# Spreading the decay rows by matmuls for four units of a gated attention, gate rows in three parts, and the exponents of two units ahead of the first product

## The reference

```python
for t in range(S):
    m_new = np.maximum(f_gate[:, :, t] + m, i_gate[:, :, t])
    f_stab = np.exp(f_gate[:, :, t] + m - m_new)
    i_stab = np.exp(i_gate[:, :, t] - m_new)
    C = f_stab * C + i_stab * outer(v_t, k_t);  n = f_stab * n + i_stab * k_t
    y[:, :, t] = sigmoid(o_t) * (C @ q_t) / np.maximum(np.abs(n @ q_t), 1.0)
x = y as (2, 768, 320)
u = x + (relu(x.T @ w_tok1) @ w_tok2).T;  x = u + relu(u @ w_ch1) @ w_ch2
gate = sigmoid(causal convolution of x with 5 taps per channel)
out = (gate * (x @ w_val)) @ w_out
```

## Time and profile before

| what | value |
|---|---|
| runs | 309.8, 310.57, 307.46 us, median 309.8 |
| span of the profiled execution, first to last instruction | 308.2 us |
| what lies around the span, taken as median less span | 1.6 us |
| busy: TensorE, VectorE, ScalarE, GpSimd | 88%, 68%, 40%, 29% |
| mean granted clock of TensorE | 0.966 |

### The profile page before, as it was taken

The page is one execution under the profiler, slowest core; times in us unless marked ns, Lnnn a source line. Parts: engine busy times, 40 slices in busy tenths (PEclk is TensorE's granted clock), DMA queues, the critical chain, the costliest instruction groups (busy, mean ns, idle before and its releaser), DMA issues.

```text
span 308.2 us, 5374 instructions
## 1 busy us (share of the span) xinstructions
PE 270.8 (88%) x2024; PEld 258.5 (84%) x2024; DVE 210.7 (68%) x415; ACT 121.9 (40%) x224; POOL 89.4 (29%) x102
## 2 busy tenths in 40 slices
PE   0876765884999999999999999999999999999854
PEld 0765654783998999999899999999999999999754
DVE  7999999977778687576677740352774138763693
ACT  4344453432874453434434223323123333231623
POOL 4537445554046445334610400000004000040340
PEclk9999598796899999999999999999999999999999
DMA  7599833344547554242000001000000010000011
GB/s 223 158 309 310 241 128 83 100 170 144 169 128 217 141 155 117 66 136 65 2 0 0 3 0 66 0 0 2 0 2 1 32 34 0 2 0 1 23 43 64
DMA packets 26289, 25.70 MB, mean 83 GB/s; under 512 B 13976, under 2 KB 22008, under 8 KB 26264
## 3 DMA queue, kind: packets, MB, share of 16 engines
q1 hardware_dynamic: 21976, 18.72, 20.9%
q10 hardware_dynamic: 4288, 6.64, 6.5%
HBM read 23.34 MB, written 2.02 MB: 82 GB/s over the span
## 4 chain that ended last, share of the span: by engine, by line
PE 60%; DVE 17%; issue 7%; ACT 6%; DMA 4%; POOL 3%; SPq 1%; ACTq 0%; DVEq 0%; POOLq 0%
PE shared L1171 25%; PE h_ps L1309 18%; DVE prob L933 7%; PE s_ps L1209 3%; DVE gate L1037 2%; PE hv_ps L1190 2%; PE shared L1274 2%; PE s_ps L1246 2%; PE hv_ps L1194 2%; PE shared L1230 2%; DVE y_lo L942 1%; DMA G_all<-G_scratch 1%; PE shared L1259 1%; DMA stage<-val 1%; DMA stage<-wout 1%
## 5 line engine op out<-in xcount | busy, mean ns | idle before, releaser
L933 DVE SCALAR_TENSOR_TENSOR prob<-G_all,A_col,mask_sb 128x128 f32<-128x128 f32 x96 | 51.3, 602 | 0.2 <-DMA G_all<-G_scratch 0.2
L1101 DVE SCALAR_TENSOR_TENSOR h_lo<-shared,h_hi 128x384 fp32r<-128x384 f32 x48 | 26.5, 557 | 35.0 <-ACT h_hi L826 34.8
L1309 PE MATMUL h_ps<-ch_hi,h_hi 128*128 128x320 f32 x144 | 45.4, 315 | 0.0
L1309 PE MATMUL h_ps<-ch_hi,h_lo 128*128 128x320 f32 x144 | 44.5, 309 | 0.0
L826 ACT ACTIVATE h_hi<-shared 128x384 fp32r<-128x384 f32 x48 | 23.1, 488 | 53.8 <-PE shared L1171 50.8
L1309 PE MATMUL h_ps<-ch_lo,h_hi 128*128 128x320 f32 x144 | 44.3, 308 | 0.0
L697 ACT ACTIVATE prob<-prob 128x512 f32<-128x512 f32 x24 | 15.0, 631 | 48.5 <-DVE prob L933 48.4
L1171 PE MATMUL shared<-u_hi,ch_hi 128*128 128x384 f32 x96 | 32.9, 342 | 0.6 <-DVE yt L982 0.4
L1171 PE MATMUL shared<-u_lo,ch_hi 128*128 128x384 f32 x96 | 32.5, 339 | 0.0
L1171 PE MATMUL shared<-u_hi,ch_lo 128*128 128x384 f32 x96 | 32.5, 338 | 0.0
L1037 DVE SCALAR_TENSOR_TENSOR gate<-x,conv_sb,gate 128x384 f32<-128x384 f32 x44 | 29.0, 668 | 1.0
(11 more groups left out here) (189 smaller groups left out, 620.6 us busy)
## 6 DMA issues: line engine op xcount, KB each, us to landing
G_all<-G_scratch SPq DMA_DIRECT2D x11, 512.0 KB, 4.8
o_sig<-on ACTq DMA_DIRECT2D x2, 960.0 KB, 6.1
k_in<-kT SPq DMA_DIRECT2D x24, 80.0 KB
q_in<-qT SPq DMA_DIRECT2D x24, 80.0 KB
kn_in<-kn SPq DMA_DIRECT2D x12, 160.0 KB, 3.9
v_in<-vn SPq DMA_DIRECT2D x12, 160.0 KB, 4.6
stage<-ch ACTq DMA_DIRECT2D x3, 640.0 KB, 4.4
out<-o_sb SPq DMA_DIRECT2D x12, 160.0 KB, 1.8
```

What stands on the lines that cost most here:

```text
L933: last = dve.scalar_tensor_tensor(out=prob[(2 * u + g) % 4][:, tile_cols(j)], in0=G_all[u % 2][:, tile_cols(h)], scalar=A_col[:, col:col + ...
L1101: took(dve.scalar_tensor_tensor(out=h_lo[i % 3][:], in0=ps_of(key)[:, 0:T], scalar=0.0, in1=h_hi[i % 3][:].bitcast(F32), op0=ALU.max, op1= ...
L1309: last = pe.matmul(h2_ps[t][:, 0:DM], a[:, tile_cols(t)], w[:, f, :], start=(f == 0 and n == 0), stop=(f == FT - 1 and n == 2))
```

## The change

Four things are done together.
- `spread(u)` on TensorE: for units 0 to 3, a matmul per head whose weights are one column of the identity, repeated 128 times, and whose data are the 16 G rows, puts the head's G row on all 128 partitions of a bank of `h2_ps`. For units 1 to 3 eight more, 64 wide, put the rows for the decays in `h2_ps[2]`. Exponents and decays of these units read PSUM. Only units 4 to 11 still go through DRAM.
- From unit 4 on `h2_ps[2]` holds a copy of the mask; the exponents of units 4 to 6 read the mask from there and G from SBUF. Units 7 to 11 read both from SBUF as before.
- The gate rows are made in three parts, chunk 0, chunk 1, and chunks 2 to 5. The third stands behind the first product on VectorE.
- The exponents of unit 1 move ahead of the first product. The buffer for `ht` is doubled, fills of buffers change engine and place, and A and W columns are copied together by VectorE.

```diff
-ROWS_PARTS = ((0, 1), (1, NC))
+ROWS_PARTS = ((0, 1), (1, 2), (2, NC))
+SPREAD = 4
...
             sp.wait_ge(pool_init, 3)
             kn_chunk(0)
             v_chunk(0)
-            sp.wait_ge(G_saved[0], 16)
...
+            sp.wait_ge(zeroed_next, 2)
+            q_chunk(1)
             k_chunk(1)
-            q_chunk(1)
-            sp.wait_ge(G_saved[1], 32)
-            G_chunk(1)
             kn_chunk(1)
             v_chunk(1)
             piece(sp, 0)
             for u in range(2, NU):
                 chunk(u)
+                if u == 2:
+                    sp.wait_ge(G_ready, 3)
+                    G_save(sp, 0, SPREAD, NC, G_saved)
+                    G_save(sp, 1, 0, NC, G_saved)
...
+                if u < SPREAD:
+                    act.wait_ge(spread_ready, u + 1)
...
+                    act.activation(decay[:], h2_ps[2][:], ACT.Exp).then_inc(decay_ready, 1)
+                    if u == SPREAD - 1:
+                        act.wait_ge(decay_ready, with_state(u))
+                        act.activation(mask_ps, mask_sb[:], ACT.Copy).then_inc(mask_ready, 1)
+                    return
...
                         last = dve.scalar_tensor_tensor(
-                            out=prob[(2 * u + g) % 4][:, tile_cols(j)], in0=G_all[u % 2][:, tile_cols(h)],
-                            scalar=A_col[:, col:col + 1], in1=mask_sb[:], op0=ALU.add, op1=ALU.min)
+                            out=prob[(2 * u + g) % 4][:, tile_cols(j)],
+                            in0=h2_ps[g][:, tile_cols(j)] if u < SPREAD else G_all[u % 2][:, tile_cols(h)],
+                            scalar=A_col[:, col:col + 1], in1=mask_ps if SPREAD <= u <= NC else mask_sb[:],
+                            op0=ALU.add, op1=ALU.min)
...
             exponents(0)
+            columns(1)
+            exponents(1)
             for n in range(ATT_STEPS):
                 attention(0, n)
+                if n == 0:
+                    gate_rows(2)
...
+            def spread(u):
+
+                pe.wait_ge(G_ready, cols_of(u))
+                if u > 0:
+                    pe.wait_ge(expo_ready, 2 * u)
+                if u > 1:
+                    pe.wait_ge(decay_ready, with_state(u - 1))
+                for h in range(H):
+                    g, j = divmod(h, HG)
+                    last = pe.matmul(h2_ps[g][:, tile_cols(j)], ident_f[0:B * H, h:h + 1].broadcast_to([B * H, P]),
+                                     G_row[:, tile_cols(u)], start=True, stop=True)
+                for j in range(HG if u > 0 else 0):
+                    for g in range(2):
+                        h = g * HG + j
+                        last = pe.matmul(h2_ps[2][64 * g:64 * g + 64, tile_cols(j)],
+                                         ident_f[0:B * H, h:h + 1].broadcast_to([B * H, 64]),
+                                         G_row[:, tile_cols(u)], start=True, stop=True)
+                last.then_inc(spread_ready, 1)
...
             pe.wait_ge(ident_ready, 1)
             columns(0)
+            spread(0)
+            columns(1)
             for n in range(ATT_STEPS):
                 attention(0, n)
-                if n == 0:
-                    columns(1)
-                else:
+                if n > 0:
                     turn_y(0, n)
+                if n == 1:
+                    columns(2)
+                if n in (1, 2):
+                    spread(n + 1)
```

More of the change, by code:

```diff
@@ L347, in with_both, with G_loads, cols_of @@
             return (NC - 2) * (u // NC) + min(u % NC, NC - 2)
+        def G_loads(u):
+            return (u - SPREAD) // 2 + 1
+        def cols_of(u):
+            n = u % NC
+            return next(k for k, (c0, c1) in enumerate(ROWS_PARTS) if c0 <= n < c1) + 1
         def k_buffer(u):
@@ L553, in _, with less_m @@
             pool.memset(v_in[2][:, :, D:D1], 1.0).then_inc(pool_init, 1)
-            for k, (c0, c1) in enumerate(ROWS_PARTS):
+            def less_m(k):
+                c0, c1 = ROWS_PARTS[k]
                 cols = slice(c0 * L, c1 * L)
@@ L675, in columns @@
             def columns(k):
[L677 to L681, removed]
-            def decays(u):
-                act.wait_ge(G_in[u % 2], 16 * (u // 2 + 1))
+                act.wait_ge(cols_copied, k + 1)
+                cols = slice(ROWS_PARTS[k][0] * B * H, ROWS_PARTS[k][1] * B * H)
+                act.activation(w_col[:, cols], w_col[:, cols], ACT.Exp).then_inc(cols_ready, 1)
+            def decays(u):
+                if u < SPREAD:
+                    act.wait_ge(spread_ready, u + 1)
+                    if with_state(u) > 1:
+                        act.wait_ge(qs_ready, with_state(u) - 1)
+                    if with_both(u - 1) > 0:
+                        act.wait_ge(kept_ready, with_both(u - 1))
+                    act.activation(decay[:], h2_ps[2][:], ACT.Exp).then_inc(decay_ready, 1)
+                    if u == SPREAD - 1:
+                        act.wait_ge(decay_ready, with_state(u))
+                        act.activation(mask_ps, mask_sb[:], ACT.Copy).then_inc(mask_ready, 1)
+                    return
+                act.wait_ge(G_in[u % 2], 16 * G_loads(u))
                 if with_state(u) > 1:
@@ L886, in _, with gate_rows @@
             dve.wait_ge(rows_init, 2)
-            for k, (c0, c1) in enumerate(ROWS_PARTS):
+            def gate_rows(k):
+                c0, c1 = ROWS_PARTS[k]
                 cols = slice(c0 * L, c1 * L)
@@ L910, in columns @@
             def columns(k):
[L911 to L914, removed]
+                full(dve, ("rows", k))
+                cols = slice(ROWS_PARTS[k][0] * B * H, ROWS_PARTS[k][1] * B * H)
+                ps = ps_of(("rows", k))[:, 0:2 * NC * B * H].rearrange("p (r x) -> p r x", r=2)
+                took(dve.tensor_copy(AW_col[:, :, cols], ps[:, :, cols]), ("rows", k))
                 done(dve, ("rows", k))
+                dve.sem_inc(cols_copied, 1)
+            gate_rows(0)
+            gate_rows(1)
             columns(0)
@@ L987, in attention @@
                 if u == 0:
-                    columns(1)
                     dve.wait_ge(apart_zeroed, 2)
-                if n + 1 < NC:
+                if u == 1:
+                    columns(2)
+                if n + 1 < NC and u > 0:
                     exponents(u + 1)
@@ L1211, in attention @@
                         last.then_inc(s_ready, 1)
+                if u == 0:
+                    spread(1)
                 if n < NC - 1:
```

69 lines of the change are left out of this document (38 added, 31 removed).

## The result

The changed kernel takes **319.8 us** (median of four runs, 319.29 to 320.58) where the kernel before takes 308.75 beside it: 1.033 times as long, 95% interval 1.027 to 1.040 (the two medians alone give 1.036, inside it). The forecast was 303.2, range 298.5 to 309.5. It is wrong in its sign.

What follows compares the result with a forecast made beforehand. The prediction took VectorE, above all the exponents contending with GpSimd, to bound the stretch before 75 us. It summed -5.0 at unit 5's product and -1.6 in the tail to -6.6: span 301.6, total 303.2 us, range 298.5 to 309.5.

Steps and rivals of the forecast that it cites:

- Exponents with a PSUM input: VectorE, units 0 to 6: one PSUM input avoids contention with GpSimd, 2.3 us a unit, bounds 2.2 and 6.5.
- the lock stays: Rival: exponents with a PSUM input wait for GpSimd all the same, 13.1 us more, total 316.3; chance 0.04.
- The round of units 4 and 5: First batch without spreads: a round of 6.2 us, exponents 5 at 53.1, product of unit 5 at 56.0 (-5.0).
- The sum for VectorE: VectorE's round from exponents 4 on: 2.3 + 0.5 + 0.1 + 1.3 + 0.3 + 1.6 = 6.1 us.
- Head and spreads: Start up to first product: 18.3 against 15.81, +2.5; spreads 1 to 3 at 3.0 us each, faster clock level.
- slow clock: Rival: TensorE stays at the slower clock level up to unit 3, 13.8 us more, total 317.0; chance 0.08.
- the prediction's own bound: Head: if TensorE stays slow throughout, spread 1 ends at 19.8 and the first product starts at 22.1.
- I find no later pause over 3 us: Argument against the slow-clock rival: TensorE works from 6 to 16 us nearly without pause, later pauses at most 3 us.
- Gate rows, part three: VectorE, between first and second product: 8.1 us, bounds 6.4 and 8.9, ending at 28.5; exponents 2 at 32.2, +7.3.
- turning its columns, 0.7: TensorE, after the third gate rows end at 28.5: 0.7 us, then spread 2 of 3.0, exponents 2 at 32.2.
- Tail: 61 to 75 us: VectorE's y goes before GpSimd's split piece and waits less, -1.6 us, bounds 0 and 3.2.
- Its sum: Exponents or products by unit: +2.5 head, +7.3 unit 2, +5.3 unit 3, +2.0 unit 4, -5.0 product 5; tail -1.6.

Runs made afterwards that it cites:

- the repeat: The changed kernel again, unedited, on a second chip beside the kernel before: 316.46 us, 1.019 (1.016 to 1.021).
- The best with the spreads: The changed kernel with gate rows moved ahead of exponents 1, state's copy on ScalarE, and G spread for units 0 and 1 only: 303.35 us, 0.976.
- the best without them: The kernel before with the mask in PSUM and the state's copy on ScalarE, no spreads or gate-row changes: 296.33 us, 0.953.
- the two cures: On the kernel before: mask in PSUM alone, 304.39 us (0.979); state's copy on ScalarE alone, 309.97 us (0.997); both, 296.33 us (0.953).
- 128-row spreads: Spread matmuls over 128 rows, 112 of them zero: on the changed kernel 313.40 us (1.009); with gate rows moved and copy on ScalarE 304.28 us (0.980).
- both kernels with 16 rows and the gate rows moved: The changed kernel with its third gate-row set ahead of exponents 1, 313.78 us (1.006); the same plus the state's copy on ScalarE, 307.00 us (0.988).

## Why the prediction was wrong

The product of unit 5 was forecast at 56.0 and came at 70.58, 14.6 us later; the span was forecast at 301.6 and came at 317.4, an error of 15.8, the rest being the tail. Step by step of the prediction:

**Exponents with a PSUM input: right.** Forecast 2.3 us a unit, measured 2.15, maximum 353 ns. The rival "the lock stays" fell, as the prediction meant it.

**The round of units 4 and 5: wrong, and no rival named the copy.** The sum for VectorE reads "2.3 + 0.5 + 0.1 + ...", and the 0.5 is the copy at its old duration. It was short because it ran behind exponents that had waited until GpSimd was through. With short exponents the copy meets GpSimd itself and measures 2.34, 2.36, 3.73 and 2.36 us. The step from exponents 4 to 5 took 8.65 instead of 6.2, that to product 5 4.45 instead of 2.9. Together that is 4.0 of the 14.6 us. Shown by moving the copy and nothing else: exponents 4 to 5 in 6.61, exponents 4 to product 5 in 8.68 instead of 13.10 (forecast 9.1). TensorE's pace (8.2 us), the bank (1.6) and the rows (0.3), told below, make 14.1 with these 4.0; the rest is spread over small terms. So by size the pace is the larger part of the miss in this execution.

**Head and spreads: the mechanism of the rival "slow clock", given 0.08.** First product at 21.21 against 18.3; the prediction's own bound, if TensorE stayed slow, was 22.1. Spread 2 at 5.7 against 3.0. Hv in unit 3's step at the slower pace, 3.3 against 2.1. Hv and scores behind spread 3 end 5.4 us after exponents 3 start, against 4.0, which made the step from exponents 3 to 4 take 7.98 instead of 6.5. These are 2.9, 2.7, 1.2 and 1.4 us, 8.2 in all. The price for the rival was 13.8 because it also had unit 3's whole round slow. The argument against it, "I find no later pause over 3 us", was false: TensorE stood still for 4.84 us from 28.5, and the granted clock fell to 0.50 in that pause, at 32.6. The forecast's own times held such a pause: with hv, scores, state and turning at its prices (1.07, 1.95, 0.76, 0.55) from 19.6, TensorE is through near 24, and the rows end at 28.5. In the repeat the head was fast and the change still lost 1.9%, with spread 2 at 3.76 as in the first run: the level of the head decides how much is lost, not whether.

**Gate rows, part three: the duration right, the dependency missed.** They took 8.4 us (forecast 8.1) and end at 31.8 (28.5 plus the late head). Then was to come "turning its columns, 0.7". The turn writes the bank "shared", and in that bank's order it stands behind the new state of unit 1, which waits for the second product, which stands behind the gate rows. It began at 33.34, 1.6 us after the rows were done, at the end of the pause of 4.84 us that the rows themselves had opened. Putting the rows into VectorE's earlier wait brought the second product from 31.69 to 26.24.

**Tail: 1.6 us forecast, 0.4 came** (the product of unit 5 is 9.6 us late, the span 9.2 longer). The y at 78.04 again starts 0.05 us behind GpSimd's split and takes 2.11. With the copy on ScalarE it did come (0.49): there ScalarE waited 1.10 us for the load, and VectorE went first.

**The price of spreading.** The prediction said that the waits for G from DRAM are not on the path, so their removal is worth nothing, and yet put the matmuls that replace them on the engine that then sets the steps. Its sum had that cost (behind the first product it stands at +2.5, by unit 3 at +5.3, head and gate rows included), but took it to be won back in units 4 and 5 by exponents that need no spread, only the mask. Mask and spread are separate parts: the mask is the part that wins, and the kernel before with mask and copy alone is 4.7% faster.

**What stays open.** The best with the spreads (303.35) is 7 us behind the best without them (296.33); in the profiles the first product stands at 21.2 and 15.7, which would carry 5.5 of it, but no run separates the head's parts. That the granted clock falls at spread 3 with 16 rows and not with 128 is seen in six profiles against two. That the rows are the reason is argued from this; how much of the 2.7 us they make, and why the head is fast in some executions of one program and slow in others, is not settled.

## What to carry to other kernels

When an instruction waits for another engine, ask which instruction behind it has the same need: freeing the first hands the wait to the next. Here the two cures were worth 5.9 and nothing alone, and 14.5 us together. And a change that replaces a load by matmuls should first show that somebody waits for that load; to split such a change into its parts costs little and found the winning one.

## What the runs showed of the hardware

- A VectorE instruction that meets GpSimd waits through a run of several GpSimd instructions without a break between them, not only for the one under way: 3.53 us over three, and the copy's 3.47 over three here.
- TensorE's pace can fall without a pause: behind 16-row spreads the scores take 2.23 to 2.56 us in six profiles, behind 128-row spreads 2.05 in two. The granted clock falls to 0.50 there in the six, between 43.8 and 50.0 us, and not in the two. In both kernels with 16 rows and the gate rows moved it fell inside spread 2 (2.69, then 1.97 where 128 rows have 1.09), and the granted clock with it, at about 30.4 us.
- The same program shows spread 1 at 3.78 and at 2.05 in two executions. A single profile of the first 20 us is no measurement of the clock there, and the granted clock reads 1.00 beside both durations.
